# A fused RWKV-style recurrence and two dense blocks: the weighing of r and k by u moves from ScalarE to GpSimd

## What is computed

```
for t in range(S):
    kt, vt, rt, wt = (k[:, :, t], v[:, :, t], r[:, :, t], w[:, :, t])
    cur = np.einsum('bhd,bhe->bhde', u[None] * kt, vt)
    y[:, :, t] = np.einsum('bhd,bhde->bhe', rt, state + cur)
    state = wt[:, :, :, None] * state + np.einsum('bhd,bhe->bhde', kt, vt)
...
h = np.maximum(xt @ w_tok1, 0.0) @ w_tok2            # over tokens, xt is x transposed
u = x + h.transpose(0, 2, 1)
h2 = np.maximum(u @ w_ch1, 0.0) @ w_ch2              # over channels
x = u + h2
...
gate_pre += conv_w[k][None, None, :] * xp[:, k:k + S, :]     # five taps along the sequence
gate = 1.0 / (1.0 + np.exp(-gate_pre))
val = x @ w_val
return (gate * val @ w_out).astype(np.float32)
```

## Time and profile before

| | |
|---|---|
| median of 3 runs | 643.46 us (641.77 to 644.45) |
| the profiled execution | 644.56 us, of which 642.5 us are the span |
| PE busy | 603.5 us (94% of the span) |
| DVE busy | 398.5 us (62%) |
| ACT busy | 217.5 us (34%) |
| POOL busy | 51.7 us (8%), 88 instructions |
| mean granted clock of PE | 0.995 of full speed |

### The profile page before, as it was taken

One profiled execution on the slowest core, in us unless ns is written; L12 is line 12 of the kernel. 1 busy time (PEld: TensorE's weight loads), 2 busy tenths in 40 slices (PEclk: granted clock), 3 DMA queues, 4 the chain that ended last, 5 costly groups with the idle time before them and its releaser, 6 DMA issues.

```text
span 642.5 us, 22783 instructions
## 1 busy us (share of the span) xinstructions
PE 603.5 (94%) x10478; PEld 581.8 (91%) x10478; DVE 398.5 (62%) x628; ACT 217.5 (34%) x407; POOL 51.7 (8%) x88
## 2 busy tenths in 40 slices
PE   3588899999999999999999999999999999999997
PEld 3577788999999999999999999999999999999997
DVE  6896576686676485686667485586666362452616
ACT  4246526135244134124244133223332131221312
POOL 0003401003001001102001000103002000000000
PEclk9999979999999999999999999999999999999999
DMA  9922624402203100401202200300000000000000
GB/s 243 244 76 70 192 82 137 125 4 67 72 3 101 38 15 15 113 2 55 85 4 76 62 1 28 114 3 3 27 3 2 26 24 2 1 1 26 2 26 24
DMA packets 13327, 35.18 MB, mean 55 GB/s; under 512 B 1584, under 2 KB 7984, under 8 KB 11888
## 3 DMA queue, kind: packets, MB, share of 16 engines
q1 hardware_dynamic: 9776, 29.01, 15.7%
q10 hardware_dynamic: 3456, 4.72, 2.1%
HBM read 29.01 MB, written 4.72 MB: 52 GB/s over the span
## 4 chain that ended last, share of the span: by engine, by line
PE 82%; DVE 6%; issue 4%; ACT 4%; POOL 2%; DMA 1%; DVEq 0%; SPq 0%; ACTq 0%; POOLq 0%
PE ps L763 82%; DVE gate L730 3%; POOL st L432 1%; DMA w<-in_w_dram 1%; POOL st L429 1%; ACT gate L547 1%; DVE rk L582 1%; DVE hid L674 1%; DVE rk_next L582 1%; DVE us L689 1%; ACT fk L465 1%; DVE ch L588 0%; ACT x2s L441 0%; ACT hid L531 0%; ACT fk L441 0%
## 5 line engine op out<-in xcount | busy, mean ns | idle before, releaser
L763 PE MATMUL ps<-us,ch 128*128 128x256 f32 x1296 | 166.9, 283 | 3.1 <-DVE us L689 2.8
L763 PE MATMUL ps<-hid,ch 128*128 128x256 f32 x1296 | 164.6, 282 | 0.0
L763 PEld LDWEIGHTS ps<-us,ch 128*128 128x128 f32 x1296 | 156.9, 188 | 6.2 <-DVE us L689 3.9
L763 PEld LDWEIGHTS ps<-hid,ch 128*128 128x128 f32 x1296 | 156.5, 188 | 1.4
L674 DVE SCALAR_TENSOR_TENSOR hid<-ps,hid 128x512 fp32r<-128x512 f32 x72 | 49.7, 690 | 122.3 <-ACT hid L531 122.3
L531 ACT ACTIVATE hid<-ps 128x512 fp32r<-128x512 f32 x72 | 42.9, 596 | 155.6 <-PE ps L763 155.3
L730 DVE SCALAR_TENSOR_TENSOR gate<-xf,cw,gate 128x256 f32<-128x256 f32 x144 | 69.7, 530 | 3.7 <-ACT gate L547 2.7
L763 PE MATMUL ps<-rk 48*64 48x32 f32 (+1 forms) x2240 | 47.2, 244 | 18.2 <-DVE rk L582 11.7
L763 PEld LDWEIGHTS ps<-rk 48*64 48x64 f32 (+1 forms) x2240 | 43.7, 163 | 22.6 <-issue 20.4
L582 DVE TENSOR_TENSOR rk<-rk,wp 112x1024 f32<-112x1024 f32 x35 | 43.1, 1233 | 21.9 <-PE ps L763 21.8
L763 PE MATMUL ps<-x2s,val 128*128 128x256 f32 x324 | 41.6, 285 | 1.6 <-DVE hid L674 1.6
(11 more groups left out here) (84 smaller groups left out, 630.2 us busy)
## 6 DMA issues: line engine op xcount, KB each, us to landing
rk<-in_rk_dram SPq DMA_DIRECT2D x7, 896.0 KB, 6.4
w<-in_w_dram SPq DMA_DIRECT2D x12, 448.0 KB, 3.6
vs<-in_v_dram SPq DMA_DIRECT2D x12, 384.0 KB, 6.6
out_dram<-gate ACTq DMA_DIRECT2D x24, 192.0 KB, 1.9
rk_next<-in_rk_dram SPq DMA_DIRECT2D x5, 896.0 KB, 6.3
gate<-in_moe_w_ch_dram SPq DMA_DIRECT2D x6, 384.0 KB, 3.1
xf<-in_moe_w_ch_dram SPq DMA_DIRECT2D x6, 384.0 KB, 3.3
gate<-in_moe_w_tok_dram SPq DMA_DIRECT2D x2, 384.0 KB, 11.4
```

The lines of the kernel that those rows point to most:

```text
L763: return nc.tensor.matmul(out, lhsT, rhs, start=start, stop=stop, skip_group_check=True, **kw)
```

## The change

`weigh` leaves ACT and goes to POOL. There it is one `tensor_tensor` multiplication of 112x1024 elements with `ut` (u, one number for each row and pair of heads) repeated along the columns, in place of four ACT operations with a scale for each row. POOL waits itself for `rk` to land and for the level 1 of the super-unit that had `fk` before. The counts of `weighed` fall from four to one for each super-unit. Nothing else changes; the plain copy stays on ACT.

```diff
         @block.gpsimd
         def _(pool):
+            def weigh(s):
+                pool.wait_ge(rk_in[landing(s)], 16 * landings(s))
+                need(pool, lev_done[1], 4 * tenant(s))
+                plain, first = rk_sides[landing(s)][0:RD, 0:1], first_rk[home(s)][0:RD, 0:1]
+                steps = [[PH * CH + 1, 2], [QS * CH, PAIRS], [2, SU // 2]]
+                scale = bass.AP(ut.tensor, ut.offset, [[ut.ap[0][0], RD], [0, 2], [1, PAIRS], [0, SU // 2]])
+                nc.gpsimd.tensor_tensor(bass.AP(first.tensor, first.offset, [list(first.ap[0])] + steps),
+                                        bass.AP(plain.tensor, plain.offset, [list(plain.ap[0])] + steps),
+                                        scale, ALU.mult).then_inc(weighed, 1)
...
+            pool.wait_ge(u_in, 16)
             for kind, n, name in PROGRAM:
-                if kind == "att" and name == "D":
+                if kind == "att" and name == "F":
+                    weigh(n)
+                elif kind == "att" and name == "D":
                     states(n)
...
         @block.scalar
-            def weigh(s):
-                for p in range(PAIRS):
-                    at, steps = p * QS * CH, [[PH * CH + 1, 2], [2, SU // 2]]
-                    plain, first = rk_sides[landing(s)][0:RD, at:at + 1], first_rk[home(s)][0:RD, at:at + 1]
-                    nc.scalar.activation(bass.AP(first.tensor, first.offset, [list(first.ap[0])] + steps),
-                                         bass.AP(plain.tensor, plain.offset, [list(plain.ap[0])] + steps),
-                                         ACT.Copy, scale=ut[0:RD, p:p + 1]).then_inc(weighed, 1)
             def att(s, name):
                 if name == "F":
                     first_operands(s)
-                    if s == 0:
-                        act.wait_ge(u_in, 16)
-                    weigh(s)
...
-                        dve.wait_ge(weighed, PAIRS * (s + 1))
+                        dve.wait_ge(weighed, s + 1)
...
-                    pe.wait_ge(weighed, PAIRS * (s + 1))
+                    pe.wait_ge(weighed, s + 1)
```

## The result

The changed kernel takes 649.48 us (median of 4 runs, 647.14 to 651.82) against 643.86 us before (median of 4 runs, 641.77 to 644.45). The medians are 5.6 us apart; the ratio of the two sets is 1.0102, 95% interval 1.0068 to 1.0136, so the kernel is slower by 4.4 to 8.8 us. The forecast was 652 us. The changed kernel's profiled execution was its fastest: 647.14 us, of which 645.1 are the span.

A forecast was written before the change was run, and what follows sets the result against it. PE was taken as the bound from 150 to 300 us, DVE from 27 to 50. Start 1.4, F:1 6.6 and F:3 0.6 sum to 8.6 us, giving 652 us; own range 648 to 655.5, whole range 645 to 657.

The forecast's parts named there:

- F:3: At F:3, twice: DVE's taps wait for POOL's weighing and `hid` stays as late or later; +0.3 us each.
- F:1: At F:1, three trips: weighing follows POOL's delayed states, so PE gets its first L1 operands late; +2.2 us each, 6.6 in all.
- the start: First 25 us: POOL's weighings hold up DVE, partly hidden behind PE's own waits; +1.4 us.
- What bounds the kernel: PE bounds 150 to 300 us, DVE 27 to 50 us; ACT's load by itself is no bound in either stretch.
- ACT's relief: Removing 48 ACT operations takes some 21.3 us off ACT's busy time; rival that this wins: 639 us, chance 0.05.
- The weighing's duration: Each POOL multiplication of 112x1024 was put at 2.4 us, with bounds of 1.8 and 3.15 us.
- Taking turns, for the whole length: POOL and two-SBUF-input DVE operations do not overlap; a long weighing can hold up DVE for up to 2.4 us.
- The rival of the turn given back: A long POOL operation lets DVE through in between; sum 0, 643.5 us, chance 0.16.
- DVE's carry finds POOL at work: At the start, DVE's carry due at 13.6 waits for POOL until 15.5, making DVE 2.7 us late.
- The fourth weighing: In the prologue, it falls behind the states of super-unit 1, where DVE has idle time, and costs nothing.
- F:2: At F:2, three times: the weighing behind D:1's states falls in DVE's idle time, with nothing in its way; 0 us.
- the four at 196.50: At F:3, DVE's four taps, two SBUF inputs each, ready at 196.50, wait 1.8 us for POOL's weighing.

The follow-up runs named there:

- the second set: The changed kernel timed again, unaltered, against the kernel before: 648.55 against 642.30 us, ratio 1.0092.
- beside_read: Against the kernel before, ACT still weighing: POOL gets two extra 112x1024 multiplications reading SBUF, results unused; one DVE operation of 0.28 us took 1.98 us.
- start_only: Changed kernel with POOL weighing only super-units 0, 1 and 2, ACT all others: 642.06 us against 641.83 us for the kernel before, ratio 1.0008.
- f1_no_relief: Changed kernel with POOL weighing only super-units 4, 7, 10 and ACT kept busy there by repeated copying: 644.95 against 642.28 us before, ratio 1.0039.
- ahead_f1: Changed kernel with the weighings of super-units 4, 7, 10 moved ahead of the states of D:0 on POOL: 644.72 against 642.30 us before, ratio 1.0035.
- only_f1_ahead: Changed kernel with POOL weighing only super-units 4, 7, 10, ahead of the states of D:0: 643.98 against 642.28 us before, ratio 1.0030.

## Why the prediction was right, and where its sizes were off

The forecast was 8.6 us. Measured were 5.6 and, in the second set, 6.2 us by the medians, and 6.6 and 5.9 us by the ratios. The forecast's own range of 648 to 655.5 us is added up a little too narrowly: with F:3 at 0.6 us its bounds for F:1 and the start give 647 to 656 us.

- *What bounds the kernel*: right. The loss is where PE waits, and ACT's relief of 19.4 us of busy time (21.3 forecast) gave nothing.
- *The weighing's duration* was set at 2.4 us and is 1.90. The term was mis-sized by taking the whole of the small multiplication but 0.1 us as work for each element; the copy's proportion, the lower bound, gave 1.8. The Trainium skill's price ("GPSIMD Engine Reference", section 3.1), 2.2 us as an estimate, was nearer and still too high.
- *Taking turns, for the whole length*: right for a long POOL operation. The rival of the turn given back has fallen, with 1.99 and 2.13 us on small DVE operations and with beside_read. It is not right for short ones: beside POOL's states the eight taps lost only 1.0 us.
- *The start*, +1.4 us: measured 0.2 us (start_only, interval -0.6 to +1.6 us). The profile of start_only has D:0 of the prologue at 53.7 us; the two of the changed kernel have 54.0 and 55.5. Its step "DVE's carry finds POOL at work" failed: at 13.01 DVE asked first. The turns came all the same, and were covered by PE's waits marked "issue", which was the lower bound. The fourth weighing, put at nothing, ends a PE wait of 0.7 us at 71.45 in the prologue (0.2 us in the second profile).
- *F:1*, 3 x 2.2 us: measured 2.7, 1.0 and 1.0, 4.7 us. The mechanism was right in both parts, and f1_no_relief shows the second one, that ACT's relief delays the states, as the larger in the second trip (0.8 of 1.23 us). The two later trips were mis-sized at three points. Against D:0 of the second trip, the weighing began 0.6 us earlier than I put it, because the states lost 1.2 us and not 1.65. It took 2.08 us instead of 2.4. And PE began to wait 0.4 us later than the 260.94 that I took, since it first did 24 matmuls of A. The first trip came out higher where the clock fell behind the wait (1.4 us where it did not). The fall of the clock was in no term of the forecast; where it came, it brought the total 1.3 us nearer to the forecast by luck.
- *F:2*, 0: right. *F:3*, +0.3: at most 0.2 us; the waits for `hid` stayed, as forecast, though it was the eighth tap of the group before that stood behind the weighing, and not the four at 196.50.
- A fixed sum of waits is not all: with the weighings moved ahead some 0.3% is left in the medians, which no wait in the profiles of ahead_f1 and only_f1_ahead explains.

## What to carry to other kernels

Ask not only how long an operation takes on the engine that it moves to, but what stands ahead of it in that engine's order: 1.9 us of work cost nothing behind D:1 and 1.0 us or more behind D:0. An engine that is relieved delivers earlier, and what it delivers can get in the way of the engine that was given the work: here that was 0.8 of the 1.23 us lost at one place. An operation on GpSimd that reads SBUF can cost a VectorE operation with two SBUF inputs all that it still has to run, however small that one is (here 1.99 us for 0.28, 2.13 for 0.42 and 1.89 for 0.17); look for places where VectorE is idle or nobody waits for it.

## What the runs showed of the hardware

A GpSimd multiplication of 112x1024 in fp32, with a step of two elements in and out and a repeated second operand, took 1.90 us, and one of 112x192 took 0.51 us: as an estimate from the two, 1.67 ns for each further element. A fill of 112x1728 took 1.55 us and held up nobody. After the same TensorE wait of 2.0 us the granted clock was 0.67 in the following stretch of one profile and 1.00 in that of another; the stretch from D:0 to D:1 was 1.3 us longer in the first.
